# Pooled attention of the undivided head pairs rearranged into quarters of TensorE's array

## The reference

```python
q_d = q.reshape(B, H, Sd, factor, D).mean(axis=3)      # factor 4, Sd = 144; k_d and v_d the same
out_d = sm_attn(q_d, k_d, v_d)                         # softmax(q_d k_d^T / 8) v_d
out_up = np.repeat(out_d, factor, axis=2)
mask = np.abs(pos[:, None] - pos[None, :]) < factor    # a band of width 7
scores = np.where(mask, scale * np.matmul(q, k.transpose(0, 1, 3, 2)), -1e9)
out_local = np.matmul(softmax(scores), v)
attn_out = out_up + out_local                          # then (B * S, H * D) = (2304, 512)
h = np.maximum(np.maximum(x @ w1, x @ w2), x @ w3)     # d_ff 768
y = h @ w_out
g = y @ w_in                                           # d_ff 2048, leaky with 0.01
return np.maximum(0.01 * g, g) @ w_out2
```

## Time and profile before

| | us |
|---|---|
| median of 3 runs (772.09 to 772.23) | 772.14 |
| the profiled execution, its own time | 771.94 |
| its span from first to last instruction | 770.2 |
| PE busy in it | 762.8 |
| DVE busy | 446.5 |
| ACT busy | 296.3 |
| POOL busy | 167.0 |

### The profile page before, as it was taken

One profiled execution on the slowest core, in us unless ns is written; L12 is line 12 of the kernel. 1 busy time (PEld: TensorE's weight loads), 2 busy tenths in 40 slices (PEclk: granted clock), 3 DMA queues, 4 the chain that ended last, 5 costly groups with the idle time before them and its releaser, 6 DMA issues.

```text
span 770.2 us, 13539 instructions
## 1 busy us (share of the span) xinstructions
PE 762.8 (99%) x5412; PEld 684.7 (89%) x5412; DVE 446.5 (58%) x769; ACT 296.3 (38%) x697; POOL 167.0 (22%) x208
## 2 busy tenths in 40 slices
PE   9999999999999999999999999999999999999998
PEld 7889989888888889999998988989898998889896
DVE  6867797666745463765756566564434466334433
ACT  4675544333242323433544354442222244222222
POOL 3795121211111333340435533110000000000000
PEclk9999999999999999999999999999999999999999
DMA  8642432332121023212567644446432236223402
GB/s 286 212 161 96 138 119 80 103 96 71 49 76 37 1 68 120 66 44 85 169 254 262 257 178 151 191 152 215 158 118 96 96 133 236 96 97 107 156 25 83
DMA packets 37630, 98.91 MB, mean 128 GB/s; under 512 B 2880, under 2 KB 23360, under 8 KB 34496
## 3 DMA queue, kind: packets, MB, share of 16 engines
q1 hardware_dynamic: 37568, 98.05, 36.4%
HBM read 73.92 MB, written 24.12 MB: 127 GB/s over the span
## 4 chain that ended last, share of the span: by engine, by line
PE 95%; DVE 2%; ACT 1%; issue 1%; DMA 1%; SPq 0%; DVEq 0%; ACTq 0%
PE mlp_ps L1067 10%; PE mlp_ps L1069 9%; PE mlp_ps L1068 9%; PE mlp_ps L1219 8%; PE mlp_ps L1221 8%; PE mlp_ps L1220 8%; PE att_ps L1240 6%; PE att_ps L1242 6%; PE att_ps L1241 6%; PE mlp_ps L1242 3%; PE mlp_ps L1241 3%; PE mlp_ps L1240 3%; PE att_ps L1139 2%; PE att_ps L1141 2%; PE att_ps L1140 2%; PE att_ps L1056 2%
## 5 line engine op out<-in xcount | busy, mean ns | idle before, releaser
L1067 PE MATMUL mlp_ps<-x_hi,wa_lo 128*128 128x288 f32 (+1 forms) x288 | 101.7, 353 | 0.1
L1069 PE MATMUL mlp_ps<-x_hi,wa_hi 128*128 128x288 f32 (+1 forms) x288 | 97.4, 338 | 0.0
L1068 PE MATMUL mlp_ps<-x_lo,wa_hi 128*128 128x288 f32 (+1 forms) x288 | 97.1, 337 | 0.0
L1507 ACT ACTIVATE h_last_a<-wa_raw 128x384 fp32r<-128x384 f32 x72 | 37.8, 524 | 104.7 <-DVE wa_raw L1841 104.1
L1067 PEld LDWEIGHTS mlp_ps<-x_hi,wa_lo 128*128 128x128 f32 x288 | 54.0, 188 | 6.0 <-DVE x_raw L1676 0.3
L1839 DVE TENSOR_TENSOR wa_raw<-mlp_ps,h_raw 128x384 f32<-128x384 f32 x24 | 13.4, 557 | 79.1 <-PE mlp_ps L1221 51.4
L1069 PEld LDWEIGHTS mlp_ps<-x_hi,wa_hi 128*128 128x128 f32 x288 | 54.1, 188 | 4.6
L1068 PEld LDWEIGHTS mlp_ps<-x_lo,wa_hi 128*128 128x128 f32 x288 | 54.3, 188 | 4.0
L1853 DVE TENSOR_TENSOR h_last_b<-wa_raw,h_last_a 128x384 fp32r<-128x384 f32 x72 | 43.3, 605 | 23.5 <-ACT h_last_a L1507 21.1
L855 POOL TENSOR_TENSOR v_rows<-v_rows 72x512 f32<-72x512 f32 x16 | 21.0, 1312 | 152.2 <-DMA v_rows<-in_v_sum 152.2
L1242 PE MATMUL att_ps<-wa_hi,h_last_a 128*128 128x512 f32 x132 | 52.2, 396 | 0.0
(11 more groups left out here) (215 smaller groups left out, 2049.1 us busy)
## 6 DMA issues: line engine op xcount, KB each, us to landing
u_even<-u_scratch SPq DMA_DIRECT2D x8, 1792.0 KB, 7.4
u_odd<-u_scratch SPq DMA_DIRECT2D x8, 1792.0 KB, 7.3
kq_in<-in_kq SPq DMA_DIRECT2D x14, 576.0 KB, 3.9
u_scratch<-u_even SPq DMA_DIRECT2D x4, 1792.0 KB, 8.7
u_scratch<-u_odd SPq DMA_DIRECT2D x4, 1792.0 KB, 9.7
v_rows<-in_v_sum SPq DMA_DIRECT2D x16, 288.0 KB
wa_raw<-in_w SPq DMA_DIRECT2D x6, 768.0 KB, 6.3
v_win<-in_v_band SPq DMA_DIRECT2D x12, 384.0 KB, 3.6
```

The costliest lines, as they stand in the source:

```text
L1067: nc.tensor.matmul(ps, wlo, xhi, start=(n == 0), stop=False)
L1068: nc.tensor.matmul(ps, whi, xlo, start=False, stop=False)
L1069: last = nc.tensor.matmul(ps, whi, xhi, start=False, stop=(n == len(pairs) - 1))
L1507: nc.scalar.activation(g_tile(0, quad, part), g_raw[part], ACT.Copy).then_inc(g_hi_ready, 1)
```

## The change

All of it concerns the whole units.

- Pooled scores: eight matmuls in place of four. Each takes 64 of the queries' columns of `kq_sum` instead of 72, in two steps c = 0 and 64, so that each fills one quarter of the array (row half = head, column half = c). Tiles of 72 queries are made of 128 columns, of which those behind the 72nd are computed and not used, and the second tile's keys are read from a place 16 columns earlier. For this `kq` is laid out anew: q first, then the last 16 groups of k, then all of k (1216 columns for 1152).
- Transposes: the probabilities of the four pieces lie side by side and are transposed in six pieces of 128 keys in place of eight of 72, all into `dt0`; ACT copies them with one instruction of 128 x 432, with the factor 1/4, in place of two of 72 x 288.
- Pooled output: 128 keys as two halves of 64, in four quarter matmuls (`pooled`), and the last 16 keys with zeros around in four small ones (`pooled_rest`), which stand between the local matmuls where two of the four quarters had nothing to do. The results lie in columns 348 to 491 of `av0` and `av1` (`UP_AT`). The banks `dt1` and `up` are no longer used by whole units.
- So the pooled output of a whole unit is in two halves: ACT copies that in `av0`, now after the whole of `av0` is done, and DVE adds that of `av1` before it combines.
- The values come by one transfer of 128 rows and four of 16 rows into 128 partitions, the rest of which POOL has cleared once (`clear_rest`, at 13.0 in the table). POOL's sums have the same free size as before.

```diff
+MAIN = P
+REST = SD - MAIN
+KQ = 2 * S + FACTOR * REST
+KQ_SUM = 2 * SD + REST
+UP_AT = 3 * BLOCKS2
...
+    put(13.0, ("C", 0))
...
+                if part == WHOLE:
+                    sums = kq_sum[:, p % PAIRS]
+                    for n, (q0, nq) in enumerate(tiles):
+                        for c in (0, TQ):
+                            for h in range(2):
+                                rows = slice(h * D, (h + 1) * D)
+                                last = nc.tensor.matmul(gs[h][c:c + TQ, n * SD:(n + 1) * SD], sums[rows, q0 + c:q0 + c + TQ],
+                                                        sums[rows, KQ_SUM - SD - n * REST:KQ_SUM - n * REST], start=True, stop=True)
...
+                    flat = prob_g[:nq, u % 2].rearrange("p i k -> p (i k)")
+                    firsts = [i * SD + (i % 2) * REST for i in range(4)] + [MAIN, 2 * SD + MAIN - P // 2]
+                    for n, first in enumerate(firsts):
+                        last = nc.tensor.transpose(bank("dt0", u)[:, n * nq:(n + 1) * nq], flat[:, first:first + P], ident[:nq, :nq])
...
+                def pooled(r, h):
+                    rows, keys = slice(h * D, (h + 1) * D), slice(r * TQ, (r + 1) * TQ)
+                    nc.tensor.matmul(bank(f"av{r}", u)[rows, UP_AT:UP_AT + SD], v_mean[keys, p % PAIRS, 0, rows],
+                                     probT_g[keys, (1 - h) * SD:(2 - h) * SD], start=True, stop=(r == h), skip_group_check=True)
+                def pooled_rest(h, n):
+                    r = 1 - h
+                    rows, keys = slice(h * D, (h + 1) * D), slice(r * TQ, (r + 1) * TQ)
+                    nc.tensor.matmul(bank(f"av{r}", u)[rows, UP_AT + n * KG:UP_AT + (n + 1) * KG],
+                                     v_mean[keys, p % PAIRS, 1, n * D:(n + 1) * D],
+                                     probT_g[keys, (4 + r) * KG:(5 + r) * KG], start=False, stop=True, skip_group_check=True)
+                if part == WHOLE:
+                    for r, h in ((0, 0), (1, 1), (0, 1), (1, 0)):
+                        pooled(r, h)
...
                     for r, h in ((0, 0), (1, 1), (0, 1), (1, 0)):
+                        if part == WHOLE and turn < 2 and r != h:
+                            pooled_rest(h, turn)
+                            continue
...
+                act.wait_ge(att_done, JOB["av0" if part == WHOLE else "up", u] + 1)
...
+                    nc.scalar.activation(upT[:, 0:nq], bank("av0", u)[:, UP_AT:UP_AT + nq], ACT.Copy).then_inc(up_evac, 1)
...
+                if part == WHOLE:
+                    dve.wait_ge(att_done, JOB["av1", u] + 1)
+                    count_step(u, "up")
+                    nc.vector.tensor_tensor(upT[:, 0:SD], bank("av1", u)[:, UP_AT:UP_AT + SD], upT[:, 0:SD], ALU.add
+                                            ).then_inc(dve_step, 1)
+                    dve.wait_ge(dve_step, step[u, "up"])
...
+            def clear_rest():
+                pool.wait_ge(vmean_ready, PAIRS)
+                nc.gpsimd.memset(v_rows[:, :, FACTOR * P:2 * FACTOR * P], 0.0).then_inc(rest_cleared, 1)
```

More of the change, by code:

```diff
@@ L255 @@
     for _kind in stage_jobs(_item):
-        if _kind in ("dt1", "lt1") and UNITS[_item[1]][1] != WHOLE:
+        if _kind == ("up" if UNITS[_item[1]][1] == WHOLE else "lt1"):
             continue
@@ L913, in _ @@
                     sums(item[1])
+                elif item[0] == "C":
+                    clear_rest()
                 elif item[0] == "W":
@@ L1002, in transposes @@
                     pe.wait_ge(probs_ready, normalised(u) - 1)
[L1003 to L1008, removed]
+                begin(("dt0", u))
+                if part == WHOLE:
[3 more added lines that the diff above has]
+                        last = nc.tensor.transpose(bank("dt0", u)[:, n * nq:(n + 1) * nq], flat[:, first:first + P], ident[:nq, :nq])
+                else:
+                    for n in range(2 * KT):
+                        kt, i = divmod(n, 2)
+                        last = nc.tensor.transpose(bank("dt0", u)[:KG, n * nq:(n + 1) * nq],
                                                    prob_g[:nq, u % 2, i, kt * KG:(kt + 1) * KG], ident[:nq, :nq])
-                        n += 1
-                    if part == WHOLE or kt == KT - 1:
-                        last.then_inc(att_done, 1)
+                last.then_inc(att_done, 1)
                 pe.wait_ge(probs_ready, normalised(u))
@@ L1027, in values @@
                 pe.wait_ge(probT_evac, EVACS[u + 1])
[L1028 to L1035, removed]
+                if part != WHOLE:
+                    begin(("up", u))
+                    ps = bank("up", u)
+                    for kt in range(KT):
+                        for h in range(2):
+                            rows = slice(h * D, (h + 1) * D)
+                            last = nc.tensor.matmul(ps[rows, 0:nq], v_mean[:KG, p % PAIRS, kt, rows],
+                                                    probT_g[:KG, (2 * kt + h) * nq:(2 * kt + h + 1) * nq],
+                                                    start=(kt == 0), stop=(kt == KT - 1))
+                    last.then_inc(att_done, 1)
                 pe.wait_ge(vwin_loaded[u % 2], 16 * (u // 2 + 1))
@@ L1275, in exps @@
                     h, tile = divmod(i, ng)
-                    last = nc.scalar.activation(prob_g[:nq, u % 2, i, :], att_ps[:nq, 2 + h, tile * SD:(tile + 1) * SD], ACT.Exp,
+                    n_i = (1 - h) * ng + tile if part == WHOLE else i
+                    last = nc.scalar.activation(prob_g[:nq, u % 2, n_i, :], att_ps[:nq, 2 + h, tile * SD:(tile + 1) * SD], ACT.Exp,
                                                 bias=bias_g[:nq, u % 2, i:i + 1], scale=SCALE / FACTOR ** 2,
-                                                accum_out=row_sum[:nq, u % 2, SLOTS + i:SLOTS + i + 1])
+                                                accum_out=row_sum[:nq, u % 2, SLOTS + n_i:SLOTS + n_i + 1])
                 last.then_inc(exp_done, 1)
@@ L1920, in laid_out @@
     return {
-        "kq": np.stack([k, q], axis=3),
-        "v_sum": groups.reshape(B, PAIRS, KG, FACTOR, KT * P),
+        "kq_parts": kq_parts,
+        "kq_whole": kq_whole.reshape(NPAIR - PAIRS, P, KQ),
+        "v_parts": groups.reshape(PAIRS, KG, FACTOR * KT * P),
+        "v_whole": v_whole[:, :, :MAIN].transpose(0, 2, 3, 1, 4).reshape(NPAIR - PAIRS, MAIN, FACTOR, P),
+        "v_rest": v_whole[:, :, MAIN:],
         "v_band": v_band.reshape(B, PAIRS, P, NV, P),
```

95 lines of the change are left out of this document (65 added, 30 removed).

## The result

The changed kernel takes 768.06 us (median of 4 runs, 767.35 to 768.94), the kernel before 772.18 beside it; the ratio is 0.9946, 95% interval 0.9929 to 0.9964. The forecast was 766.5 with a range of 764.9 to 769.5: faster, as forecast, and inside the range, 1.6 us above the forecast time. It is outside the 765.7 to 767.4 that the forecast allowed itself, and in the 767.5 to 769 of rival 5. The profiled execution is the slowest of the four, 768.94 us with a span of 767.2 (before: 770.2).

A forecast was written before the change was run, and what follows sets the result against it. PE, busy 99%, bounds the kernel. Savings of 1.35 (scores), 3.65 (values) and 1.25 (transposes) make 6.25, less 0.66 for DVE's add: 5.6 us. From 771.94 that gives 766.3, as median 766.5; range 764.9 to 769.5.

The forecast's parts named there:

- rival 5: A wait put at nothing shows in some units, 0.1 to 0.3 us in each of ten: 767.5 to 769; chance 0.10.
- Scores, values, transposes: PE's savings per whole unit in pooled scores, values stage and transposes: 0.15, 0.365 and 0.125, together 0.64 us.
- Rival 1: Transposes: 128-column weights set the pace, 0.11 us each, 0.285 a unit more than forecast: 769.4; chance 0.12.
- rival 2: Values: 72-column quarter passes don't run beside 58-column ones, four more rounds, 0.24 us in ten units: 768.9; chance 0.08.
- rival 3: Scores and values: four quarters at 144 columns run only two at a time: 774.7, slower than before; chance 0.05.
- The tight places: Transposes of units 9 and 10, where PE waits for DVE's combining: savings lost, 0.33 us more in each.
- the add's 0.33 on top: DVE's extra 128 x 144 instruction in each combine, 0.33 us; costs PE at units 9 and 10, 0.66 together.
- Rival 4: DVE has room after all in the transposes of units 9 and 10: 764.6; chance 0.07.
- The 48 more transfers of values and their wait for the clearing: SP's queue: issued five dense groups ahead of the values' use, so they cost nothing.

## Why the prediction was right, and where it was off

- **Scores, values, transposes.** 0.15, 0.365 and 0.125 a unit; measured 0.15, 0.36 and 0.12, and 1.31 to 1.40 for the scores part by undoing it. Rival 1 (0.11 for each transpose with 128 columns of weights), rival 2 and rival 3 are out: six in 0.38, the local part of the values in 0.82, four rounds of four quarters in the 0.55 of the pooled scores. By the Trainium skill's rule (TensorE: Matmul & The Clock Gate, LDWEIGHTS (loading the stationary operand)) the six would have taken 0.64; the measurement decides against it for transposes one behind the other.
- **The tight places.** Savings lost and the add's 0.33 on top, in each. The add cost 0.33 and 0.32 (shown by leaving it out), the net was 0.27. Rival 4 (DVE has room) is out. That DVE was full, as I wrote, is only half of it: the order on DVE and ACT put a dense group first, and two moves in it, together with that of POOL's sums, won 2.6 us at the end of the attention and 2.0 in the median.
- **The step that failed** is "The 48 more transfers of values and their wait for the clearing stand in SP's queue five dense groups ahead of the use; POOL's sums keep their size. Nothing." Both are true as far as the values' use goes. What I did not ask is what POOL's sums run beside: DVE's `h_lo`, with PE right behind it. At the values of unit 7 it cost 0.55 to 0.60 in each profile of the changed kernel, because the sum starts later relative to DVE. A second term was too small in the same way: the add's "0.33 on top" was counted only up to the transposes, but it also puts `h_lo` behind the next sum, which cost 0.43 ahead of the scores of unit 13 and went when the add was left out. Some 0.9 to 1.1 came back both by shrinking the sums and by moving them. This is rival 5, a wait put at nothing, but in two places and not in each of ten units. The row that could have told it stands in the trace of before: `h_lo` at 70.79 with 0.74 for 0.45. There it cost PE next to nothing, as the step of -0.03 with tiny sums shows.
- **The rest** of the 1.6 us: without those two steps the profile after would have been 4.5 sooner at the end of the attention, and the front part of that one execution lost 1.26 more, which two other profiles did not. The three medians of the changed kernel, 767.5 to 768.1, are 1.0 to 1.6 above the forecast; the two collisions explain 1.0 of that. Against the kernel before beside them they are 4.1, 5.4 and 5.2 faster, where 5.6 was forecast, so how near the forecast came depends on the group. That the first median lies inside the range is in part owed to the room that the range had for other rivals. Why a weight transfer lands late in some executions stays open: ACT's wait for it, 1.10 to 1.31, stands in four profiles of the changed kernel and its variants and not in the single one of the kernel before, and no experiment was made on it.

## What to carry to other kernels

When an edit makes a transfer land later, or puts an instruction in front of an engine's others, list what the moved work will now run beside, and not only whether its result is in time; here PE lost 1 us because DVE twice came behind a POOL instruction that nobody waited for. Where an engine seems full at a tight place, look at the order of its queue before giving the place up: ask which of its next instructions PE needs first, and then follow the wait, which moved twice here before it went. And read the price of a stage from the next start: the prices of scores and values held to 0.01 in all twelve units, that of the transposes in the ten without a wait.

## What the runs showed of the hardware that I had not expected

- **DVE against POOL.** DVE's add or subtraction of two SBUF sources (128x288, usually 0.45) took 1.50, 1.46, 1.43 and 1.32 beside a POOL addition of 1.28 or 1.29 that began 0.10 to 0.27 earlier, 1.11 where POOL's had begun 0.48 earlier (with the scores part undone, at 119.79) and 0.74 where it had begun 0.87 earlier. Each time it ended some 0.31 behind POOL's. It goes the other way round too: where `h_lo` began first, at 106.18 without the add, it took 0.45 and POOL's sum, from 106.29, took 1.48. The Trainium skill (SBUF — State Buffer, 🔬 SBUF: two separate sides) calls the pair of ports that both use "an **exclusive lock**, not a bandwidth split", for DVE instructions with two SBUF inputs against POOL ones that read SBUF; these traces agree. With one source in PSUM there is no stretching: in the kernel with the sums moved, DVE's 128x640 instruction with `att_ps` and `mask` took 0.81 beside POOL's sum (80.88 to 82.16), and 0.81 in the changed kernel, where POOL idled.
- **Quarters take work by themselves.** Passes for the two free quarters started 0.01 behind the small ones of the other two, ahead of small ones that precede them in the code. An order by turns was worth 0.06 in a stage, not 0.24.
- **The clock in the front part.** In three of the experiments' profiles (POOL's sums tiny, POOL's sums moved, small matmuls in rounds of their own) the granted clock fell to 0.50, the lower level of 1.2 GHz, right behind PE's wait around 21 us. Windows of the kernel with POOL's sums moved (stretch; its length, then busy time of PE, weight loads, DVE, ACT, POOL; clock, DMA share, GB/s):

```profile
20.00:22.00 2.00, 0.40 (x4) 0.41 (x5) 1.48 (x3) 1.54 (x4) 2.00 (x3) 0.95 0.29 100
22.00:24.00 2.00, 2.00 (x11) 1.88 (x9) 1.73 (x4) 1.49 (x6) 2.00 (x5) 0.50 0.04 17
24.00:26.00 2.00, 2.00 (x36) 1.64 (x36) 1.30 (x4) 2.00 (x7) 2.00 (x3) 0.70 0.03 8
```

PE had been busy 0.40 of the 2 us before. In the same 2 us it was busy 0.66 in the first profile of the changed kernel, whose clock stayed at its full value, and 0.72 with tiny sums, where the clock fell all the same (0.72 from 22 to 24, 0.50 from 24 to 26). From the transposes of unit 1 (21.60) to the dense work (28.06) this profile fell from 0.26 to 1.49 behind the first one of the changed kernel: some 1.2 of the 2.14 that it had lost ahead of the scores of unit 8.
